# FFT filter and mixture of experts on one core: the way back's first matmuls as two 64x128 tiles in place of four 64x64 tiles

## What is computed

```python
def _attn_ref(x, filt_r, filt_i):
    X = np.fft.rfft(x, axis=1)
    F = (filt_r + 1j * filt_i)[None, :, :]
    Y = X * F
    return np.fft.irfft(Y, n=x.shape[1], axis=1).astype(np.float32)

def _moe_ref(x, w_gate, w1, w2, capacity):
    logits = x @ w_gate
    expert_idx = np.argmax(logits, axis=1)
    ...                       # softmax weight of the chosen expert
    if counts[e] < capacity:  # first come, first served, cap = N // E * 2
        disp[e, counts[e]] = x[i]
    ...
    h = np.maximum(np.einsum('ecd,edf->ecf', disp, w1), 0.0)
    y = np.einsum('ecf,efd->ecd', h, w2)
    out[i] = gate_w[i] * y[expert_idx[i], pos[i]]   # rows kept; the others stay zero
```

## Time and profile before

| | us |
|---|---|
| Median of 3 runs | 488.03 (487.88 to 489.23) |
| Profiled execution, its own time | 487.66 |
| Span of the profiled execution, first to last instruction | 485.8 |
| PE busy | 456.1 (94%) |
| PEld busy | 401.8 (83%) |
| DVE busy | 230.2 (47%) |
| ACT busy | 215.3 (44%) |
| Granted TensorE clock, mean | 0.996 of full speed |

### The profile page before, as it was taken

How to read it: one execution, slowest core, us unless ns; L and a number is a source line. 1 busy time by engine, 2 the same in 40 slices (tenths; PEclk the granted TensorE clock), 3 DMA queues, 4 the chain that set the end, 5 groups by cost and what they waited for, 6 DMA issues and landing times.

```text
span 485.8 us, 12483 instructions
## 1 busy us (share of the span) xinstructions
PE 456.1 (94%) x5352; PEld 401.8 (83%) x5352; DVE 230.2 (47%) x376; ACT 215.3 (44%) x402; POOL 185.9 (38%) x159
## 2 busy tenths in 40 slices
PE   5989999998789879999999999999999999999993
PEld 5865557665666575999989999999999999999993
DVE  2086537995679666771472143354124344214300
ACT  2745554633254647621654334445435345423310
POOL 0000000000000041367638787757785548584122
PEclk9999999999999999999999999999999999999998
DMA  8994999846946564932222894410894310970011
GB/s 302 409 405 130 338 277 322 284 163 216 351 144 203 195 214 149 301 100 83 72 88 65 298 375 152 153 45 22 295 400 162 120 55 24 354 263 23 32 36 37
DMA packets 45744, 93.01 MB, mean 191 GB/s; under 512 B 5840, under 2 KB 20848, under 8 KB 45168
## 3 DMA queue, kind: packets, MB, share of 16 engines
q1 hardware_dynamic: 39408, 79.48, 46.9%
q0 software_dynamic: 6272, 12.65, 7.8%
HBM read 46.47 MB, written 45.64 MB: 190 GB/s over the span
## 4 chain that ended last, share of the span: by engine, by line
PE 69%; DVE 3%; issue 2%; ACT 1%; POOLq 0%; ACTq 0%
PE psum L1306 28%; PE psum L1292 26%; PE psum L508 3%; PE psum L565 2%; PE psum L599 2%; PE psum L663 2%; PE psum L491 2%; PE psum L555 1%; DVE w1l L1041 1%; DVE hot_lo L945 1%; PE psum L575 1%; DVE prod L811 0%; PE psum L625 0%; ACT w1h L1031 0%; PE psum L595 0%
## 5 line engine op out<-in xcount | busy, mean ns | idle before, releaser
L1119 DVE SCALAR_TENSOR_TENSOR hl<-psum,hh 128x384 fp32r<-128x384 f32 x128 | 69.5, 555 | 143.5 <-ACT hh L1070 143.4
L1306 PE MATMUL psum<-w2h,hh 128*128 128x256 f32 x384 | 109.8, 286 | 0.0
L1306 PE MATMUL psum<-w2h,hl 128*128 128x256 f32 x384 | 108.6, 283 | 0.0
L1306 PE MATMUL psum<-w2l,hh 128*128 128x256 f32 x384 | 108.6, 283 | 0.0
L1070 ACT ACTIVATE hh<-psum 128x384 fp32r<-128x384 f32 x128 | 62.1, 492 | 59.6 <-PE psum L1292 59.4
L1292 PE MATMUL psum<-xh,w1h 128*128 128x384 f32 x256 | 86.1, 336 | 1.8 <-DVE hl L1119 1.4
L1292 PE MATMUL psum<-xh,w1l 128*128 128x384 f32 x256 | 85.6, 334 | 0.0
L1292 PE MATMUL psum<-xl,w1h 128*128 128x384 f32 x256 | 85.6, 334 | 0.0
L811 DVE TENSOR_TENSOR prod<-psum,fab 128x1024 f32<-128x1024 f32 x48 | 56.5, 1219 | 56.4 <-PE psum L491 41.7
L1207 POOL DMA_INDIRECT out<-o_out,token x48 | 48.9, 1019 | 68.2 <-ACT o_out L1079 53.2
L1306 PEld LDWEIGHTS psum<-w2l,hh 128*128 128x128 f32 x384 | 73.6, 192 | 0.0
(11 more groups left out here) (116 smaller groups left out, 526.8 us busy)
## 6 DMA issues: line engine op xcount, KB each, us to landing
out<-zero SPq DMA_DIRECT2D x24, 1024.0 KB, 13.0
w_raw<-in_w SPq DMA_DIRECT2D x14, 1024.0 KB, 5.7
x_in<-in_x SPq DMA_DIRECT2D x18, 512.0 KB, 6.9
t_scratch<-t_out SPq DMA_DIRECT2D x24, 256.0 KB, 4.3
z_in<-t_scratch SPq DMA_DIRECT2D x32, 192.0 KB, 5.5
y_rows<-y SPq DMA_DIRECT2D x12, 512.0 KB, 3.3
fab<-in_fab SPq DMA_DIRECT2D x4, 1024.0 KB, 14.3
first_raw<-in_w SPq DMA_DIRECT2D x2, 1024.0 KB, 9.0
```

The lines of the kernel that those rows point to most:

```text
L1119: nc.vector.scalar_tensor_tensor(out=hl[:, b % 2, f, :], in0=ps[(2, 3, 6, 7)[f % 4]][:, 0:TOK], scalar=0.0, in1=hh[:, b % 2, f, :].bitcast ...
L1306: mm = nc.tensor.matmul(ps[4 + (b * ST + s) % 2][:, 0:D], hx[:, b % 2, f, s * P:(s + 1) * P], wt[k][:, f, :], start=(f == 0 and m == 0), s ...
```

## The change

In `pe_inverse` the loop over `low` goes. One matmul has as its stationary operand all 128 channels of the half h (a 64x128 piece of `prod`), and writes all 128 partitions of `back[q]`. The moving operand, the banks, the columns in them, the terms and their order, the flags and the semaphore at the end are the same. A call has 16 or 24 matmuls in place of 32 or 48, that is 32 or 48 records of each kind. No other line changes, and the instructions of the other engines and the order of everything else on PE are as before.

```diff
                     for i, (f, c, to) in enumerate(terms):
-                        for low in range(2):
-                            for q in range(2):
-                                d = h * P + low * A1
-                                at = (h * 2 + a) * 2 * HR
-                                mm = nc.tensor.matmul(back[q][part(low), at:at + 2 * HR], prod[part(q), n % 2, f, a, c, d:d + A1],
-                                                      wbi[part(q), j, a, to, :], start=(i == 0), stop=(i == len(terms) - 1))
+                        for q in range(2):
+                            at = (h * 2 + a) * 2 * HR
+                            mm = nc.tensor.matmul(back[q][:, at:at + 2 * HR], prod[part(q), n % 2, f, a, c, h * P:(h + 1) * P],
+                                                  wbi[part(q), j, a, to, :], start=(i == 0), stop=(i == len(terms) - 1))
             mm.then_inc(bi_done, 1)
```

## The result

| | before | changed |
|---|---|---|
| Median, us | 488.27 (8 runs, 486.61 to 489.23) | 490.73 (8 runs, 489.87 to 492.80) |
| Profiled execution, us | 487.66 | 489.87 |
| Span, us | 485.8 | 488.0 |
| PE records of the way back | 1728 | 864 |

The changed kernel takes 1.006 times as long, with a 95% interval of 1.0037 to 1.0084; by the medians it is 2.5 us slower. The sign is as forecast; the forecast of 495.2 us was 7.2 us above the time before, nearly three times too much.

What follows compares the result with a forecast made beforehand. PE's own instruction stream was taken as the bound. The profiled 487.66 us + 13.1 (rounds and call ends) - 1.4 (hidden in DVE waits) - 4.5 (code gaps) gave 494.9, forecast as a 495.2 us median; range 486.5 to 501 us.

Steps and rivals of the forecast that it cites:

- What bounds the kernel, and the pace now: PE's own stream is the bound; L508's rounds take 82.5 ns, set by streaming 96 columns, with weight loads hidden.
- Term 1, the rounds: In L508, the 128-column weight load sets the pace at 111.6 ns: +29.1 ns over 432 rounds, +12.6 us.
- Term 2, the ends: At each call's ends, a longer first weight load and last matmul add 20 ns a call, +0.5 us.
- Term 3, what is hidden: In sequences 1 and 2, growth of group 6's inverse falls into PE's 1.71 us wait for DVE: -1.4 us.
- Term 4, the code: PE's "issue" gaps are waits for instruction blocks; of 6.9 us, 4.5 go; bounds 0 to -6.9 us.
- the prediction's own signs: Instruction queue with about 37 packets; PE "issue" gaps summing to 2 to 3 us, largest inside L555, third stage.
- the first case: Load-bound rounds in L508, the forecast itself: 495.2 us, from 492.8 to 499.7 with the code bounds; chance 0.76.
- the case of no change: L508's weight load takes about 92 ns, so slower rounds and code savings cancel: 487 to 489 us; chance 0.06.
- serial loads: The two tiles' weight loads in L508 exclude each other, a round takes 223 ns: 538.5 us; chance 0.04.
- streaming-bound rounds: Streaming still sets L508's round at 82.5 ns, only code savings remain: 483.8 us as a median; chance 0.14.
- the case in between: L508's weight load takes about 92 ns and the two opposing terms cancel: 487 to 489 us; chance 0.06.

Runs made afterwards that it cites:

- experiment 1: Kernel before with only the two 64x64 tiles of the low channels in all calls but the first; 478.20 us, ratio 0.9796.
- experiment 8: Changed kernel with 48 moving columns in place of 96 in all calls but the first; 1190.27 us, as other sequences ran too.
- 9: Kernel before with the third stage's z loads spread behind stores of y on SP's queue and zeros moved; 487.25 us, ratio 0.9991.
- experiment 7: Changed kernel with 16 small matmuls (64 instructions) ahead of PE's first work, moving the block borders; 492.99 us, ratio 1.0101.
- experiment 5: Kernel before, unchanged, run again for a second profile; 487.43 us, ratio 0.9981.
- experiment 6: Kernel before with zeros moved: four behind the first stores of y, two at 136 us, three behind the stages; 485.97 us, ratio 0.9947.
- 11: Kernel before with wide 64x128 tiles only in the second sequence's last call and all of the third; 486.86 us, ratio 0.9984.
- experiment 3: Kernel before with seven writes of zeros moved: five to the stores of y, two behind the stages; 487.70 us, ratio 1.0007.

## Why the prediction was wrong

*What bounds the kernel, and the pace now.* Right. PE's own stream is the bound, and the round of 82.5 ns is streaming: half the tiles pass at the same pace (experiment 1).

*Term 1, the rounds.* Right. 111.6 ns a round were forecast and 111 measured, and halving the columns streamed leaves the round at 111 (experiment 8). A load of 128 columns takes as long on 64 rows as on 128.

*Term 2, the ends.* Right within 0.5 us: from start to start a call grew by 0.47 and 0.72 us, forecast 0.49 and 0.72, so 18 x 0.47 + 6 x 0.72 = 12.8 us in place of 13.1.

*Term 3, what is hidden.* Right: each of the two waits for DVE shrank by 0.66 us, -1.3 us in place of -1.4. So rounds cost 11.5 us on the path. (Laid beside experiment 1, the calls of the changed kernel, waits taken off, add up to 11.4 us.)

*Term 4, the code.* This is the step that failed. Its mechanism stands: blocks of some 256 instructions, late where data is in front (9), with borders that can be moved (7), and gone as gaps with half the instructions (1). What remains, forecast at 2.4 us in L555 of the third stage, was 1.68, 1.81 and 1.29 us there, and PE falls back by 2.01, 2.14 and 1.62 us at it; in two of the three profiles another 0.51 and 1.01 us go in L553 of the second stage, of which the prediction had nothing. By the prediction's own signs this term looked right (one gap in L555, 37 packets); the failure lies in what no visible gap shows. What was mis-sized is what the kernel before loses: 6.9 us by the idle times, 9.1 us by the stretch of experiment 1 (136.15 against 145.21), 9.3 by the second profile (145.50). Of the missing 2.2 us, 1.8 are at the gaps themselves, where PE falls back by 0.15 to 0.39 us more than the idle time says. Most of that is, by an estimate, in how an idle time is counted: it starts at the modelled end of the last matmul, for L508 some 246 ns after its start, while the next would have started about 20 ns after it. Another 0.28 us is a delay that shows as no gap at all, in the 96 records of L555 at 74.12 us in the first profile, which last 3.10 us and 2.83 where the code is in time. About 0.2 us are spread over the calls, some 0.01 us each, and 0.15 us go the other way, a wait for DVE that only experiment 1 has. In some executions a fall of the clock is added (5, 6, 9). So the term, forecast at -6.9 + 2.4 = -4.5, was about -9.2 + 2 = -7.2 us.

Sum anew: 487.66 + 11.5 - 7.2 = 492.0 us by the profiles, +4.3. The stretches give +3.5 (148.73 - 145.21), by the later profiles +3.9 (149.36 - 145.50), and the last call, behind the stretch, adds 0.4 (from its start to the next L555 are 2.53 us before and 2.97 now), which is no more than profiles of one kernel differ behind it: from the start of the last call to the end of the span the changed kernel's three take 312.8 to 313.4 us, the kernel before 312.7. The profiled execution of the changed kernel came to 489.87 because its stages began 1.4 us earlier (26.43 against 27.84). I don't put that down to the change: with four tiles the profiles have starts of 26.6 to 28.1 us, with two of 26.3 to 27.3, and the ranges overlap. The medians say +2.5, +4.0 and +3.5; what they leave unexplained of +4.3, 0.3 to 1.8 us, is of the size of their own scatter.

The bounds of term 4, 0 and -6.9 us, were the second mistake: I took the sum of the visible gaps for the most that could come back. With -9.1 as the end, the first case would have begun at 490.6 us in place of 492.8. The whole range, 486.5 to 501 us, held the time only because it reached down to the case of no change; that was luck and not the mechanism. Of the rivals, serial loads and streaming-bound rounds are refuted by the 111 ns, and so is the case in between (a load of 92 ns), though its 487 to 489 us lie nearer to the result than the forecast. The chance of 0.8 for slower by more than 0.3% was well placed.

## What to carry to other kernels

Where a tile gets wider, compare the weight load per tile with the streaming per tile before counting instructions: fewer, wider tiles with 96 columns to stream turned a hidden load into the pace. Where PE issues an instruction every 20 to 30 ns next to heavy data traffic, the number of instructions is itself a cost, to be sized by a variant with the same pace of the array and fewer instructions, not by adding up idle times. Data moved out of the way of one block of code gets in the way of another; ask who requests what at the place where it arrives.

## What the runs showed of the hardware

- PE's instructions come in blocks of some 256, 16 KB each, on a queue of their own, and a late block stood PE still for up to 3.07 us (experiment 6). Leaving out half of the way back's instructions gave 9.1 us of the stages back (experiment 1).
- A weight load of 128 fp32 columns sets a pace of 111 ns, on 64 rows in two tiles side by side (experiment 8) as on 128 rows in one.
- The granted clock fell to half in the stages of four profiles (experiment 8 left aside): behind an idle time of PE of 2.12 us (experiment 5), 3.07 (6) and 2.70 (9), and behind one of 1.71 us alone (11). In the first profile, idle times of 1.71 and 2.43 us left it at 1.00, and in experiment 3 of 1.71 and 3.19 us. What decides isn't shown here.
- At the very start, matmuls with 128 columns of weights follow at 213 ns, and from about 11 to 13 us on at 111 (experiment 7). The ratio is near that of the clock's two levels; the profile's clock column reads 1.00 on both sides of the step, so that it is the clock isn't shown.

The Trainium skill, "TensorE: Matmul & The Clock Gate", section "LDWEIGHTS (loading the stationary operand)", has the load go by columns alone, whatever the rows: an estimate from its figure is 107 ns for 128 columns in either shape. Experiment 8, with 111 ns a round where 48 columns are streamed, agrees within 4 ns. The Trainium skill, "Runtime: NRT & Kernel Launch", section "Instruction fetch mechanics", calls the cost of crossing a 16 KiB boundary "mostly hidden"; experiment 1, with 9.1 us given back, and the gap of 2.43 us beside a DMA queue at 91 to 101% disagree for this kernel.
